# The 64-token tail of the gate's v: high and low part as one stationary factor, 8 matmuls for 12

## Chip, cores and metric

The kernel runs on one core of one Trainium2 chip. The metric is the device time of one execution in microseconds. Three runs of the kernel before gave 655.53, 655.45 and 653.43 us; their median is 655.45.

## What is computed

Three layers follow each other, for a batch of 4, 576 tokens and 512 channels, all in float32:

- attention with 8 heads of 64, each query seeing itself and the 63 keys before it;
- a gated layer: `h = relu(x @ w_in)` with `w_in` of 512 x 1024, split by columns in `u` and `v` of 512 each; `v` normalised per token, mixed over tokens by `w_spatial` (576 x 576), plus a bias, times `u`, then `@ w_out`;
- a mixer: `h = relu(xt @ w_tok1) @ w_tok2` over the tokens, added to x, then `u + relu(u @ w_ch1) @ w_ch2` over the channels, with `w_ch1` of 512 x 1536.

What matters here is the second layer's v:

```python
h = np.maximum(x @ w_in, 0.0)
u, v = (h[..., :d_ff // 2], h[..., d_ff // 2:])
mu = np.mean(v, axis=-1, keepdims=True)
var = np.mean((v - mu) ** 2, axis=-1, keepdims=True)
v_n = (v - mu) / np.sqrt(var + 1e-06)
```

## The kernel before, in words

**Products in three parts.** TensorE multiplies fp32r data, a float32 rounded to fewer bits. To keep the precision every factor is held twice: a high part (the rounded value, written by ScalarE, GpSimd or VectorE into an fp32r tile) and a low part (the value minus its high part). `product` (L1289) then issues three matmuls into one accumulation: high x high, high x low, low x high. The first factor of `pe.matmul` is the stationary one, the second the moving one. `xhl[:, s, k, token]` holds x, transposed, high (s=0) and low (s=1) for the four groups k of 128 channels; `w_in_s[:, s, k, :]` holds w_in.

**Tiles of tokens.** 576 tokens are four tiles of 128 (t = 0 to 3) and a tail of 64 (t = 4). In `gate_values` (L1396) the tokens' x is the stationary factor, 128 columns wide for a tile and 64 for the tail, and 512 columns of w_in move: 4 groups x 3 products = 12 matmuls for each tile, and 12 for the tail as well. `gate_inputs` (u) and `mix_tokens` (g) move 288 columns, half of the tokens, and have eight units each per batch.

**From a finished v.** `relu_v` (L816) on ScalarE takes the ReLU from PSUM into `vr`, which has two halves used in turn, so that tile t shares its half with tile t - 2 and waits for the low part of that tile. `stats` (L1062), `spread` on GpSimd (L693) and `norm` (L1073) normalise it there, `vn_high` (L823) and `normalised_lo` (L1084) write high and low part for the mixing. Of the tail, the low part lies in partitions 64 to 127 of the high part's place, so that the mixing over 64 tokens takes two matmuls instead of three; place 4 of the low half of `vn` is free.

**Banks.** Units v, u, g, y, t, a, b and w take four PSUM banks in turn, the one used longest ago first (L158 to L178). `take_acc` (L1365) waits until the last user's result has been read (`unit_free`, L435): for v, u and y that is a ScalarE operation, for the others one of VectorE.

**Orders.** Every engine and SyncE's queue of transfers works through a list written out by hand, and each is in order. A list has a prologue (attention of batch 0), a first, two equal loops (attention of batches 1 to 3, with the second and third layer of the batch before) and an epilogue. In the list of TensorE Q, K, Z are transposes of q, k and the tail of both, S scores, T transposes of the probabilities, V attention's product with v, w transposes of w_spatial, v, u, g, y the gated layer, t, a, b the token mixer, P the first products of the last layer; "+" is the second half of the unit opened last. ScalarE's `vr`, `vh` are ReLU and high part of v, `uu` the ReLU of u, `e` the exponentials, `o` attention's output; VectorE's `vs`, `vn`, `vl` are statistics, norm and low part; GpSimd's `n` normalises probabilities, `xh`, `xl` split x, `xo`, `ao`, `wo` form low parts for the last layer. SyncE's `lq`, `lk`, `lv`, `lz` load q, k, v and the tail of q and k, `lw` the weights (0: w_in for v, 1: w_in for u, 2: w_spatial, 3: w_out, 4: w_tok1, 5: w_tok2, 6: bias). Loads of q and k go round three slots, so the seventh waits until the fourth slot's transposes are done; v has three places in batch 0, and lv03 waits until V1 is done.

## Time and profile before

| | us |
|---|---|
| median of three runs (lowest, highest) | 655.45 (653.43, 655.53) |
| the profiled execution | 653.59 |
| its span, first to last instruction | 651.0 |
| busy: TensorE / VectorE / ScalarE / GpSimd | 638.4 / 433.1 / 297.8 / 138.4 |
| mean clock granted to TensorE, of full speed | 1.000 |

The page counts an engine as busy while an instruction of its datapath runs. Matmuls overlap: one lasts longer than the distance at which the next one starts, so their price is read from starts, not from durations. In the rows below PE is TensorE, DVE VectorE, ACT ScalarE, POOL GpSimd and SPq the transfers that SyncE issues. "128\*64 128x512" is a matmul with 128 rows and 64 columns of stationary factor and 512 moving columns. In brackets stands the idle time before a group and what ended it; a timeline merges neighbours of one line, and names the shape of the first.

### The profile page before, as it was taken

What the parts mean: (1) busy time and instruction counts of PE and PEld (TensorE: products, weight loads), DVE (VectorE), ACT (ScalarE), POOL (GpSimd) and SP (SyncE); (2) the same over time, 40 slices, a digit from 0 to 9 for tenths busy, and PEclk for the clock granted to TensorE, in tenths of its full rate; (3) what the DMA queues carried; (4) which work ended last, traced back from release to release, by engine and by line L of the source; (5) the groups of instructions that cost most, each with busy time, mean ns of one, the idle gap of its engine ahead of it and who ended that gap; (6) DMA issues with size and microseconds to landing.
All of it is one profiled execution on the core that took longest, in us unless ns stands there. A gap on an engine that the chain in (4) does not pass through costs nothing.

```text
span 651.0 us, 11538 instructions
## 1 busy us (share of the span) xinstructions
PE 638.4 (98%) x3917; PEld 589.1 (90%) x3917; DVE 433.1 (67%) x1073; ACT 297.8 (46%) x733; POOL 138.4 (21%) x232
## 2 busy tenths in 40 slices
PE   5899999999999999999999999999999999999997
PEld 5798999989998899988999989988898889889886
DVE  4988887666865778766473666776756775755534
ACT  4865447334464344652347334453334454243331
POOL 3561426531234304252107700000000000000000
PEclk9999999999999999999999999999999999999999
DMA  9858135586444883344730174252632332422412
GB/s 209 212 92 197 35 86 158 129 169 107 128 117 116 178 139 87 107 121 113 165 128 2 61 177 134 73 173 83 213 108 65 121 107 64 163 64 66 162 33 97
DMA packets 190872, 77.48 MB, mean 119 GB/s; under 512 B 127328, under 2 KB 177056, under 8 KB 190816
## 3 DMA queue, kind: packets, MB, share of 16 engines
q1 hardware_dynamic: 190816, 76.76, 45.2%
q8 instruction: 32, 0.52, 0.3%
q14 instruction: 24, 0.20, 0.1%
HBM read 55.49 MB, written 21.23 MB: 118 GB/s over the span
## 4 chain that ended last, share of the span: by engine, by line
PE 95%; DMA 2%; DVE 1%; POOL 1%; SPq 0%; issue 0%; ACT 0%; POOLq 0%; DVEq 0%
PE ps L1291 71%; PE ps L1392 13%; PE ps L1361 4%; PE ps L1331 4%; DMA early<-in_moe_w_spatial_dram 2%; PE ps L1455 1%; PE ps L1310 0%; PE ps L1380 0%; DMA out_dram<-front 0%; DVE front L1195 0%; PE ps L1341 0%; DVE att L995 0%; ACT att L763 0%; POOL att L675 0%; SPq L544 0%
## 5 line engine op out<-in xcount | busy, mean ns | idle before, releaser
L1291 PE MATMUL ps<-arena 128*128 128x288 f32 (+3 forms) x2100 | 396.3, 342 | 0.0
L1291 PEld LDWEIGHTS ps<-arena 128*128 128x128 f32 (+1 forms) x2100 | 335.2, 186 | 33.7
L1291 PE MATMUL ps<-att_r,arena 128*128 128x384 f32 x504 | 101.5, 336 | 0.0
L1291 PEld LDWEIGHTS ps<-att_r,arena 128*128 128x128 f32 x504 | 90.0, 188 | 7.1
L1392 PE MATMUL ps<-arena 128*128 128x288 f32 (+1 forms) x560 | 89.6, 316 | 0.0
L1392 PEld LDWEIGHTS ps<-arena 128*128 128x128 f32 x560 | 80.5, 188 | 4.1
L690 POOL TENSOR_SCALAR att<-att,rinv 128x128 f32<-128x128 f32 x144 | 53.8, 393 | 98.1 <-DVE rinv L1006 97.9
L783 ACT ACTIVATE att<-att,nmax 128x128 f32<-128x128 f32 x144 | 56.0, 392 | 25.8 <-DVE nmax L995 25.3
L881 ACT ACTIVATE xT<-ps 128x384 f32<-128x384 f32 x54 | 26.5, 491 | 52.1 <-PE ps L1291 52.1
L1171 DVE TENSOR_TENSOR arena<-front,arena 128x1792 fp32r<-128x1792 f32 x16 | 32.4, 2025 | 16.1 <-ACT arena L873 16.0
L1181 DVE TENSOR_TENSOR vr<-ps,xT 128x384 f32<-128x384 f32 x36 | 20.0, 556 | 31.7 <-PE ps L1291 25.0
L995 DVE CUSTOM_DVE_ANT_0 att<-ps,mask 128x128 f32<-128x128 f32 x144 | 33.1, 285 | 11.5 <-PE ps L1331 11.0
L893 ACT ACTIVATE arena<-vr 128x384 fp32r<-128x384 f32 x36 | 18.7, 520 | 43.8 <-PE ps L1291 35.7
L1331 PE MATMUL ps<-att 128*128 128x128 f32 x288 | 37.4, 280 | 0.9 <-DVE att L969 0.9
L1361 PE MATMUL ps<-att 128*128 128x128 f32 x288 | 37.1, 276 | 0.7 <-DVE att L969 0.4
L873 ACT ACTIVATE arena<-front 128x1792 fp32r<-128x1792 f32 x18 | 30.7, 1704 | 13.4 <-DVE front L1161 13.4
L1186 DVE SCALAR_TENSOR_TENSOR arena<-vr,arena 128x384 fp32r<-128x384 f32 x36 | 21.2, 589 | 23.3 <-ACT arena L893 23.3
L1331 PEld LDWEIGHTS ps<-att 128*128 128x128 f32 x288 | 35.4, 196 | 1.3 <-DVE att L969 1.2
L1361 PEld LDWEIGHTS ps<-att 128*128 128x128 f32 x288 | 34.7, 192 | 1.7 <-DVE att L969 0.6
L793 ACT ACTIVATE xT<-ps 64x256 f32<-64x256 f32 x72 | 27.1, 377 | 14.6 <-PE ps L1361 13.6
L893 ACT ACTIVATE arena<-xT 128x384 fp32r<-128x384 f32 x18 | 9.5, 525 | 48.4 <-PE ps L1291 32.7
L1129 DVE TENSOR_TENSOR uy<-ps,uy 128x288 f32<-128x288 f32 x32 | 14.2, 454 | 20.4 <-PE ps L1291 20.3
(101 smaller groups left out, 651.8 us busy)
## 6 DMA issues: line engine op xcount, KB each, us to landing
front<-in_moe_w_ch_dram SPq DMA_DIRECT2D x18, 512.0 KB, 4.7
prob_blocks<-att SPq DMA_DIRECT2D x27, 256.0 KB, 2.5
att<-prob_blocks SPq DMA_DIRECT2D x108, 64.0 KB, 2.0
u_scratch<-uy SPq DMA_DIRECT2D x16, 288.0 KB, 2.9
front<-in_moe_w_ch_dram SPq DMA_DIRECT2D x18, 256.0 KB, 2.9
front<-in_moe_w_ch_dram SPq DMA_DIRECT2D x36, 128.0 KB, 3.5
early<-u_rows SPq DMA_DIRECT2D x18, 256.0 KB, 5.6
att<-in_v_dram SPq DMA_DIRECT2D x16, 256.0 KB, 3.8
```

The costliest lines, as they stand in the source:

```text
L690: ins = pool.tensor_scalar(x, x, rinv[:, g % 3, p:p + 1], 1.0, ALU.mult, ALU.mult)
L783: ins = act.activation(x, x, ACT.Exp, bias=nmax[:, g % 3, p:p + 1], scale=-1.0, accum_out=psums[:, g % 3, p:p + 1])
L793: ins = act.activation(xT3[c, :, blk * WINDOW:(blk + 1) * WINDOW], tp[c, bank, :].rearrange("p (w h n) -> p w h n", w=PAIRS, h=2)[:, :, h, ...
L873: act.activation(a_hi_at[n % 2], a_raw[n % 2], ACT.Copy).then_inc(a_hi, 1)
L881: act.activation(part[x], ps[:, 6, 0:CK], ACT.Copy).then_inc(part_copied, 1)
L893: act.activation(h_at[:, j, 0], total[i], ACT.Relu).then_inc(h_hi, 1)
L995: ins = dve.tensor_tensor_reduce(out=prob[:, g % 3, P * p:P * (p + 1)], in0=ps[:, 4 + g % 2, P * p:P * (p + 1)], in1=mask[:, 0:P] if blk e ...
L1171: dve.tensor_tensor(a_lo_at[n % 2], a_raw[n % 2], a_hi_at[n % 2].bitcast(F32), ALU.subtract).then_inc(a_low, 1)
L1291: ins = pe.matmul(dst, w[a], x[c], start=first and n == 0, stop=last and n == 2, skip_group_check=True)
L1331: ins = pe.matmul(ps[:, 4 + g % 2, P * p:P * (p + 1)], qd[:, g // 2 % 2, g % 2, p].rearrange("p h n -> p (h n)"), kT[:, p, at:at + P], sta ...
L1361: ins = pe.matmul(tp[:, bank, P * p:P * (p + 1)], window[:, P * p:P * (p + 1)], keys[:, p], start=True, stop=True)
L1392: ins = pe.matmul(dst, d, w, start=t == 0 and n == 0, stop=t == NT - 1 and n == len(pairs) - 1, skip_group_check=True)
```

## The change

For the tail, high and low part of x are written beside each other a second time, into `xtail` (128 columns: 64 high, 64 low, at the free place 4 of `vn`). One matmul with these 128 columns against the high part of w_in gives high x high in PSUM rows 0 to 63 and low x high in rows 64 to 127; a second one with the 64 high columns adds high x low to rows 0 to 63. That is 8 matmuls for 12. ScalarE copies rows 64 to 127 to `vtail` in SBUF (`tail_low`, "vt4", on the bytes of `xtail`, which has been read by then), VectorE adds them to rows 0 to 63 and writes `vr` (`tail_sum`, "va4"), ScalarE takes the ReLU in place. The bank is free after `tail_sum`. The engines that split x write `xtail` as well: ScalarE and VectorE in batch 0, GpSimd in the others. All lists of orders are replaced; those that matter below are shown, the list of SyncE with its first lines.

```diff
 ...
     PROLOGUE_PE = (
-        "Q0 K0 Q1 S0 S1 K1 K2 S2 Q2 T0 S3 V0 T1 S4 S5 T2 V1 K3 Q3 V2 T3 S6 S7 V3 T4 w0 w1 v0 Z4 w2 V4 S8 T5 + V5 "
-        "T6 v1 + w3 T7 V6 v2 + u00 V7 T8 + u10 + u20 V8 + u30 + v3 + w4 v4 + u01 w5 + u11 + u21 + u31 +").split()
+        "Q0 K0 Q1 S0 S1 K1 K2 S2 Q2 T0 S3 T1 V0 S4 S5 T2 V1 K3 Q3 T3 V2 S6 S7 V3 T4 w0 v0 w1 Z4 V4 w2 S8 T5 + V5 "
+        "T6 w3 v1 + V6 T7 v2 + u00 V7 T8 + u10 + u20 + V8 u30 + v3 w4 + v4 + u01 + u11 w5 + u21 + u31 +").split()
 ...
     LOOP_PE = (
-        "g00 S0 S1 + g10 S2 S3 + g20 + g30 + g01 + g11 + g21 + g31 S4 S5 V0 V1 + y00 + y10 + y20 + y30 + y01 S6 "
-        "V2 t0 + y11 + y21 + y31 + t1 S7 V3 t2 S8 V4 t3 t4 a0 a1 a2 a3 v0 a4 V5 V6 + v1 + b00 b10 b20 b30 b01 b11 "
-        "V7 V8 b21 v2 + b31 v3 + v4 + u00 + u10 + u20 + u30 + u01 + u11 + u21 + u31 +").split()
+        "g00 S0 S1 + g10 + S2 S3 g20 + g30 + g01 + g11 + g21 + g31 + y00 S4 V0 V1 + y10 + y20 + y30 + y01 S5 V2 "
+        "t0 S6 + y11 + y21 + y31 + S7 t1 V3 t2 t3 t4 S8 V4 a0 a1 a2 v0 a3 a4 V5 V6 + v1 + b00 b10 b20 b30 b01 V7 "
+        "V8 b11 b21 b31 v2 + v3 + v4 + u00 + u10 + u20 + u30 + u01 + u11 + u21 + u31 +").split()
 ...
     EPILOGUE_PE = (
-        "g00 + g10 + g20 + g30 + g01 + g11 + g21 + g31 + y00 + y10 + y20 + y30 + y01 + t0 t1 y11 + y21 + y31 + a0 "
-        "t2 t3 a1 t4 a2 a3 a4 P0 P1 b00 P2 b10 P3 b20 P4 b30 b01 P5 b11 P6 b21 b31").split()
+        "g00 + g10 + g20 + g30 + g01 + g11 + g21 + g31 + y00 + y10 + y20 + y30 + y01 t0 t1 + y11 + y21 + y31 + a0 "
+        "t2 t3 P0 P1 a1 t4 a2 a3 a4 P2 P3 P4 b00 b10 b20 b30 P5 b01 b11 b21 P6 b31").split()
 ...
     LOOP_ACT = (
-        "e0 e1 e2 gh00 gh10 gh20 e3 gh30 gh01 e4 gh11 yy00 o0 o1 yy10 yy20 gh21 gh31 yy30 o2 yy01 th0 e5 yy11 e6 "
-        "yy21 yy31 th1 th2 o3 th3 e7 o4 e8 th4 ah0 o5 ah1 vr0 o6 vr1 vh0 o7 o8 vr2 vh1 vr3 vh2 uu00 vr4 vh3 uu10 "
-        "uu20 uu30 uu01 uu11 vh4 uu21 uu31").split()
+        "e0 e1 gh00 gh10 e2 gh20 gh30 gh01 gh11 e3 e4 yy00 yy10 yy20 gh21 gh31 o0 yy30 e5 yy01 o1 yy11 th0 yy21 "
+        "e6 yy31 th1 o2 th2 th3 e7 th4 o3 e8 o4 ah0 o5 o6 ah1 vr0 vr1 o7 vh0 o8 vr2 vh1 vt4 vh2 vr3 uu00 vr4 uu10 "
+        "vh3 uu20 uu30 vh4 uu01 uu11 uu21 uu31").split()
 ...
     EPILOGUE_DVE = (
-        "sa00 sm00 gl00 sa10 sm10 gl10 sa20 sm20 sa30 gl20 as0 sm30 xs0 gl30 sa01 sa11 sm01 gl01 sm11 sa21 gl11 "
-        "sa31 xs1 sm21 sm31 xs2 gl21 gl31 as1 xs3 tl0 tl1 tl2 tl3 tl4 al0 al1 te00 cs0 te10 dh0 te20 te30 te01 "
-        "cs1 te11 dh1 dh2 cs2 te21 te31 dh3 ut0 ut1 ut2 ut3").split()
+        "xs0 sa00 sa10 sm00 sm10 gl00 sa20 gl10 sm20 as0 sa30 xs1 gl20 sa01 sm30 sm01 gl30 sa11 sm11 gl01 sa21 "
+        "xs2 sm21 gl11 sa31 sm31 gl21 gl31 xs3 tl0 tl1 as1 tl2 tl3 tl4 cs0 al0 al1 dh0 cs1 te00 te10 dh1 te20 "
+        "te30 te01 dh2 te11 te21 cs2 te31 dh3 ut0 ut1 ut2 ut3").split()
 ...
     EPILOGUE_POOL = (
-        "xo0 xo1 ao0 xo2 xo3 ao1 xo4 xo5 xo6 wo0").split()
+        "xo0 ao0 xo1 xo2 xo3 xo4 wo0 xo5 ao1 xo6").split()
 ...
     LOOP_DVE = (
-        "qt0 qt1 qt2 m0 qt3 m1 qt4 m2 r0 qt5 r1 sa00 pt0 sa10 sm00 sm10 pt1 gl00 gl10 sa20 r2 sm20 sa30 m3 gl20 "
-        "sa01 sm30 sm01 m4 gl30 r3 sa11 pt2 sm11 gl01 sa21 gl11 sa31 sm21 sm31 pt3 qt6 vo1 gl21 r4 gl31 m5 pt4 m6 "
-        "tl0 qt7 r5 vo2 qt8 tl1 r6 pt5 tl2 m7 pt6 m8 r7 tl3 tl4 vo3 r8 pt7 al0 pt8 al1 vs0 te00 te10 te20 vo4 "
-        "te30 te01 vn0 vs1 te11 vl0 te21 te31 vn1 ut0 vs2 ut1 vl1 vn2 vs3 vl2 vn3 ut2 ut3 vs4 kt0 vl3 vn4 kt1 vl4").split()
+        "qt0 qt1 qt2 m0 qt3 m1 qt4 r0 m2 r1 pt0 sa00 sm00 sa10 qt5 gl00 sm10 pt1 sa20 gl10 sa30 sm20 sm30 gl20 "
+        "sa01 gl30 r2 sm01 sa11 m3 sm11 gl01 pt2 sa21 gl11 m4 sa31 r3 sm21 qt6 sm31 vo1 r4 pt3 gl21 gl31 m5 qt7 "
+        "pt4 vo2 r5 m6 tl0 qt8 m7 pt5 tl1 r6 tl2 pt6 tl3 m8 vo3 tl4 r7 r8 pt7 pt8 al0 al1 vs0 vn0 te00 te10 te20 "
+        "vo4 te30 vs1 te01 te11 te21 vl0 te31 ut0 ut1 vs2 vn1 vn2 ut2 vl1 kt0 vl2 va4 vs3 kt1 vn3 vs4 ut3 vn4 vl3 "
+        "vl4").split()
 ...
     ALL_SP = (
-        "lq00 lk00 lq01 lv00 lv01 lk01 lq02 lk02 lw01 lq03 lk03 lv02 lw00 lw02 lz04 lv03 lk10 lv04 lq10 lw06 lv10 "
-        "lw03 lv11 lw04 pw10 pr10 pw11 pr11 pw12 pr12 lw05 lv12 pw13 pw14 pr13 pr14 lv13 pw15 pw16 pr15 pr16 lv14 "
 ...
+        "lq00 lk00 lq01 lv00 lk01 lv01 lk02 lq02 lw01 lq03 lv02 lk03 lw00 lw02 lv03 lz04 lw04 lv04 lk10 lw06 lw03 "
+        "lq10 lv10 pw10 pr10 lv11 pw11 pr11 pw12 lw05 pr12 lv12 pw13 pw14 pr13 pr14 pw15 lv13 pw16 pr15 pr16 pw17 "
 ...
@@ -257,6 +258,12 @@
         vn = region("vn").rearrange("p (s t n) -> p s t n", s=2, t=NT)
 
 
+        VT = START["vn"] - START["w_out"] + (2 * NT - 1) * G
+        vtail = early[0:TAIL, VT:VT + G]
+
+        xtail = vn[:, 1, NT - 1, :].rearrange("p (k s n) -> p k s n", k=KD, s=2)
+
+
         def raw(name, n, k):
             at = START[name] - START["w_out"]
             return early[:, at:at + n].rearrange("p (k n) -> p k n", k=k)
@@ -349,6 +356,7 @@
         w2_hi = sem("w2_hi")
         w2_lo = sem("w2_lo")
         a_low = sem("a_low")
+        tail_copied = sem("tail_copied")
         w2_low = sem("w2_low")
         xc_low = sem("xc_low")
         xc_in = [sem(f"xc_in{i}") for i in range(2)]
@@ -414,7 +422,7 @@
 
 
         ACC_ACT = counts(ACT_ORDER, ("vr", "uu", "yy"))
-        ACC_DVE = counts(DVE_ORDER, ("sa", "tl", "al", "te", "wl"))
+        ACC_DVE = counts(DVE_ORDER, ("sa", "tl", "al", "te", "wl", "va"))
         TP_ACT = counts(ACT_ORDER, ("qe", "ze", "o"))
         TP_DVE = counts(DVE_ORDER, ("ke", "c"))
         K_TURNED = counts(DVE_ORDER, ("kt",))
@@ -434,6 +442,8 @@
 
         def unit_free(u):
             kind, b, x = u
+            if (kind, x) == ("v", NT - 1):
+                return acc_dve, ACC_DVE["va", b, x]
             if kind in ("v", "u", "y"):
                 return acc_act, ACC_ACT[{"v": "vr", "u": "uu", "y": "yy"}[kind], b, x]
             return acc_dve, ACC_DVE[{"g": "sa", "t": "tl", "acc_a": "al", "b": "te", "w": "wl"}[kind], b, x]
@@ -701,10 +711,16 @@
                 apart(pool)
                 pool.wait_ge(*unit_full(("y", b - 1, 31)))
                 apart(pool)
+                if t == NT - 1:
+                    apart(pool)
+                    pool.wait_ge(*unit_free(("v", b - 1, t)))
+                    pool.tensor_scalar(xtail[:, :, 0, :], xT3[:, :, toks(t)], 1.0, 1.0, ALU.mult, ALU.mult)
                 pool.tensor_scalar(xhl[:, 0, :, toks(t)], xT3[:, :, toks(t)], 1.0, 1.0, ALU.mult, ALU.mult).then_inc(x_hi_pool, 1)
 
             def x_low(b, t):
                 pool.wait_ge(x_hi_pool, NT * (b - 1) + t + 1)
+                if t == NT - 1:
+                    pool.tensor_tensor(xtail[:, :, 1, :], xT3[:, :, toks(t)], xhl[:, 0, :, toks(t)].bitcast(F32), ALU.subtract)
                 pool.tensor_tensor(xhl[:, 1, :, toks(t)], xT3[:, :, toks(t)], xhl[:, 0, :, toks(t)].bitcast(F32), ALU.subtract) \
                     .then_inc(x_lo_pool, 1)
 
@@ -796,6 +812,8 @@
 
             def x_high(t):
                 act.wait_ge(*use_free("V", 0, last_blk(t)))
+                if t == NT - 1:
+                    act.activation(xtail[:, :, 0, :], xT3[:, :, toks(t)], ACT.Copy)
                 act.activation(xhl[:, 0, :, toks(t)], xT3[:, :, toks(t)], ACT.Copy).then_inc(x_hi, 1)
 
             def spatial_hi(t):
@@ -813,8 +831,19 @@
                                          ACT.Copy)
                 ins.then_inc(sp_hi, 1)
 
+            def tail_low(b):
+
+                if b > 0:
+                    act.wait_ge(*unit_free(("v", b - 1, NT - 1)))
+                act.wait_ge(*unit_full(("v", b, NT - 1)))
+                act.activation(vtail, ps[TAIL:P, BANK_OF["v", b, NT - 1], :], ACT.Copy).then_inc(tail_copied, 1)
+
             def relu_v(b, t):
                 n, r = NT * b + t, rows(t)
+                if t == NT - 1:
+                    act.wait_ge(*unit_free(("v", b, t)))
+                    act.activation(vr[0:r, n % 2, :], vr[0:r, n % 2, :], ACT.Relu).then_inc(acc_act, 1)
+                    return
                 if n >= 2:
                     act.wait_ge(vn_lo, n - 1)
                 act.wait_ge(*unit_full(("v", b, t)))
@@ -905,6 +934,8 @@
                     x_high(x)
                 elif kind == "wh":
                     spatial_hi(x)
+                elif kind == "vt":
+                    tail_low(b)
                 elif kind == "vr":
                     relu_v(b, x)
                 elif kind == "vh":
@@ -1026,6 +1057,8 @@
 
             def x_low(t):
                 dve.wait_ge(x_hi, t + 1)
+                if t == NT - 1:
+                    dve.tensor_tensor(xtail[:, :, 1, :], xT3[:, :, toks(t)], xhl[:, 0, :, toks(t)].bitcast(F32), ALU.subtract)
                 dve.tensor_tensor(xhl[:, 1, :, toks(t)], xT3[:, :, toks(t)], xhl[:, 0, :, toks(t)].bitcast(F32), ALU.subtract) \
                     .then_inc(x_lo, 1)
 
@@ -1059,10 +1092,17 @@
                                             w_sp_s[:, 0, 0:NT - 1, toks(t)].bitcast(F32), ALU.subtract)
                 ins.then_inc(acc_dve, 1)
 
+            def tail_sum(b):
+                n, bank = NT * b + NT - 1, BANK_OF["v", b, NT - 1]
+                dve.wait_ge(vn_lo, n - 1)
+                apart(dve)
+                dve.wait_ge(tail_copied, b + 1)
+                dve.tensor_tensor(vr[0:TAIL, n % 2, :], ps[0:TAIL, bank, :], vtail, ALU.add).then_inc(acc_dve, 1)
+
             def stats(b, t):
                 n, r = NT * b + t, rows(t)
                 i = n % 2
-                dve.wait_ge(*unit_free(("v", b, t)))
+                dve.wait_ge(acc_act, ACC_ACT["vr", b, t])
                 dve.bn_stats(vst[0:r, i, :], vr[0:r, i, :]).then_inc(stats_done, 1)
                 dve.wait_ge(stats_done, n + 1)
                 apart(dve)
@@ -1215,6 +1255,8 @@
                     x_low(x)
                 elif kind == "wl":
                     spatial_lo(x)
+                elif kind == "va":
+                    tail_sum(b)
                 elif kind == "vs":
                     stats(b, x)
                 elif kind == "vn":
@@ -1401,6 +1443,12 @@
                     if b == 0 and t == 0:
                         apart(pe)
                         pe.wait_ge(*piece_lo("v", i))
+                    if t == NT - 1:
+
+                        pe.matmul(acc, xtail[:, i].rearrange("p s n -> p (s n)"), w_in_s[:, 0, i, G:FF], start=i == 0, stop=False, skip_group_check=True)
+                        ins = pe.matmul(acc[0:TAIL, :], xhl[:, 0, i, toks(t)], w_in_s[:, 1, i, G:FF], start=False, stop=i == KD - 1,
+                                        skip_group_check=True)
+                        continue
                     ins = product(acc[0:rows(t), :], [xhl[:, s, i, toks(t)] for s in range(2)],
                                   [w_in_s[:, s, i, G:FF] for s in range(2)], i == 0, i == KD - 1)
                 if part == 1:
```

## Rows read from the trace of the kernel before

**Rows 1.** The page: busy time of the engines, and the granted clock in 40 slices
```profile
PE 638.4 (98%) x3917; PEld 589.1 (90%) x3917; DVE 433.1 (67%) x1073; ACT 297.8 (46%) x733; POOL 138.4 (21%) x232
...
PEclk9999999999999999999999999999999999999999
```

**Rows 2.** Windows of the start and of the last layer: busy us (instructions), clock, DMA share, GB/s
```profile
10.00:30.00 20.00, 16.29 (x129) 14.39 (x128) 17.63 (x83) 16.20 (x65) 9.77 (x22) 1.00 1.01 253
360.00:644.00 284.00, 284.00 (x1431) 256.02 (x1430) 177.41 (x270) 114.54 (x173) 9.82 (x5) 1.00 0.34 107
```

**Rows 3.** The chain that ended last: start us, us, engine and line, count
```profile
38.60 2.78 PE ps L1291 x12
```

**Rows 4.** Groups by line and shape, TensorE: count, busy us, mean ns
```profile
L1291 PE MATMUL ps<-arena 128*64 128x512 f32 x48 | 11.7, 393 | 0.0
```

**Rows 5.** Timeline of TensorE, three short looks at batch 3: start us, us, count
```profile
306.61 0.61 PE L1291 MATMUL ps<-arena 128*128 128x512 f32 x2
...
307.07 0.40 PE L1291 MATMUL ps<-arena 128*64 128x512 f32 x1
...
309.83 0.42 PE L1291 MATMUL ps<-arena 128*128 128x288 f32 x2
```

**Rows 6.** Groups by line and shape, ScalarE and VectorE, 64 partitions by 512
```profile
L821 ACT ACTIVATE vr<-ps 64x512 f32<-64x512 f32 x4 | 2.3, 587 | 3.5 <-PE ps L1291 1.8 <-DVE arena L1087 1.7
...
L1118 DVE TENSOR_TENSOR arena<-ps,arena 64x512 fp32r<-64x512 f32 x4 | 2.7, 684 | 5.5 <-ACT arena L849 5.5
```

**Rows 7.** Timeline of TensorE in batch 3, from b21 to the mixing
```profile
299.88 22.83 PE L1291 MATMUL ps<-arena 128*128 128x288 f32 x144
322.54 1.74 PE L1392 MATMUL ps<-arena 128*128 128x288 f32 x12
```

**Rows 8.** Timelines in batch 3: ScalarE after u31, VectorE's low part of tile 2
```profile
322.82 0.41 ACT L834 ACTIVATE uy<-ps 128x288 f32<-128x288 f32 x1 [1.19 <-PE ps L1291]
...
310.48 0.68 DVE L1087 TENSOR_TENSOR arena<-vr,arena 128x512 fp32r<-128x512 f32 x1
```

**Rows 9.** Timeline of GpSimd in batch 3: high and low part of the tail
```profile
302.54 0.41 POOL L704 TENSOR_SCALAR arena<-xT 128x256 fp32r<-128x256 f32 x1
303.03 0.73 POOL L708 TENSOR_TENSOR arena<-xT,arena 128x256 fp32r<-128x256 f32 x1
```

**Rows 10.** Timeline of TensorE at the start: T4, w0 with w1, Z4
```profile
29.07 0.66 PE L1341 MATMUL ps<-ident,att 128*128 128x128 f32 x4
30.05 1.09 PE L1380 MATMUL ps<-ident,early 128*128 128x128 f32 x8 [0.33 <-DMA early<-in_moe_w_spatial_dram]
...
32.37 0.60 PE L1310 MATMUL ps<-ident,att 128*128 128x128 f32 x4
```

**Rows 11.** Timeline of SyncE's queue at the start: issue us, us
```profile
15.66 0.37 SPq L530 DMA_DIRECT2D att<-in_k_dram  x1
16.07 0.58 SPq L539 DMA_DIRECT2D att<-in_v_dram  x1
...
19.54 1.41 SPq L527 DMA_DIRECT2D att<-in_k_dram  x1
22.71 2.04 SPq L539 DMA_DIRECT2D att<-in_v_dram  x1
```

**Rows 12.** DMA issues at 18.2 and 19.5 us: KB, us to landing
```profile
early<-in_moe_w_spatial_dram SPq DMA_DIRECT2D x1, 144.0 KB, 11.8
...
att<-in_k_dram SPq DMA_DIRECT2D x1, 128.0 KB, 11.4
```

**Rows 13.** Timelines at the last layer's start: GpSimd's low parts, then TensorE
```profile
346.44 3.64 POOL L721 TENSOR_TENSOR att_r<-att,att_r 128x768 fp32r<-128x768 f32 x2 [30.87 <-DVE att L1151]
350.02 4.08 POOL L728 TENSOR_TENSOR arena<-front,arena 128x1792 fp32r<-128x1792 f32 x1
...
353.15 1.64 PE L1392 MATMUL ps<-arena 128*128 128x512 f32 x6
...
358.73 2.27 PE L1291 MATMUL ps<-att_r,arena 128*128 128x384 f32 x12
```

More of the change, by code:

```diff
@@ L62, in bass_attention_gmlp_mixer_kernel @@
-        "y11 + S6 V2 t0 y21 + t1 S7 y31 + a0 t2 t3 V3 S8 t4 V4 v0 a1 a2 a3 a4 + V5 V6 b00 b10 b20 b30 v1 + b01 "
-        "b11 b21 V7 V8 v2 + b31 v3 + v4 + u00 + u10 + u20 + u30 + u01 + u11 + u21 + u31 +").split()
+        "g00 + g10 S0 + g20 + S1 S2 g30 + g01 S3 + g11 + g21 + g31 + y00 V0 S4 S5 + y10 + y20 + y30 + y01 V1 S6 "
+        "t0 t1 + y11 V2 + y21 + y31 + a0 t2 t3 V3 S7 t4 V4 S8 a1 a2 a3 v0 a4 + V5 V6 b00 b10 b20 v1 + b30 b01 b11 "
+        "V7 v2 V8 + b21 b31 v3 + v4 + u00 + u10 + u20 + u30 + u01 + u11 + u21 + u31 +").split()
@@ L76, in bass_attention_gmlp_mixer_kernel @@
-        "yy21 th1 yy31 o2 th2 th3 o3 th4 o4 e7 e8 ah0 ah1 vr0 vh0 o5 vr1 o6 o7 o8 vr2 vh1 vr3 vh2 vr4 uu00 uu10 "
-        "vh3 vh4 uu20 uu30 uu01 uu11 uu21 uu31").split()
+        "gh00 e0 gh10 e1 e2 gh20 gh30 e3 gh01 gh11 yy00 yy10 yy20 o0 gh21 gh31 yy30 e4 th0 o1 yy01 th1 e5 yy11 "
+        "yy21 yy31 e6 th2 o2 o3 th3 o4 e7 th4 e8 ah0 ah1 o5 o6 vr0 vr1 o7 vh0 o8 vr2 vh1 vr3 vt4 vh2 vr4 vh3 uu00 "
+        "uu10 uu20 vh4 uu30 uu01 uu11 uu21 uu31").split()
     LOOP_ACT = (
-        "e0 e1 e2 gh00 gh10 gh20 e3 gh30 gh01 e4 gh11 yy00 o0 o1 yy10 yy20 gh21 gh31 yy30 o2 yy01 th0 e5 yy11 e6 "
```

24 lines of the change are left out of this document (11 added, 13 removed), and 16 rows, old and new, of tables (ALL_SP, FIRST_DVE).

## Prediction

> **What bounds the kernel now.** I read the page first: TensorE is busy for 638.4 of 651.0 us, VectorE for 433.1, and the clock granted to TensorE is 9 tenths of full speed or more in all forty slices [rows 1]. A busy share alone does not settle it, since matmul ends are modelled, so I looked for gaps stage by stage: from 360 to 644 us the engine is busy for 284.0 of 284.0 us, from 10 to 30 us for only 16.29 of 20 [rows 2]. TensorE is full from about 34 us until its last products, and the only stretch with air in it is the start. That gives two rules. A matmul removed after 34 us is worth its full spacing. A changed order on another engine is worth nothing there, unless it makes TensorE wait; at the start it can shift the whole kernel either way.
>
> **The price of a matmul.** Twelve 128-wide matmuls over 512 columns advance the chain by 2.78 us, 0.232 each [rows 3]. Do those whose stationary factor has only 64 columns go faster? There are 48, the tail's twelve in each of four batches, 393 ns long on average [rows 4]. In batch 3 two 128-wide ones start at 306.61, the tail's twelve run from 307.07 on, and at 309.83 the 288-column ones begin: 0.46 / 2 = 0.230 before the tail and 2.76 / 12 = 0.230 in it [rows 5]. The spacing follows the moving columns, not the width of the stationary factor. So a factor of 128 columns costs no more than one of 64 did, and 8 matmuls take 1.84 us for 2.76.
>
> **Part 1, the removal.** (12 - 8) x 0.230 = 0.92 us per batch, times 4 batches: **-3.7 us**, all of it on the path. The weight loads that go too count as nothing: they lie beside the matmuls.
>
> **Part 2, ScalarE's copy and VectorE's sum.** ScalarE gets one more operation per batch, a 64x512 copy out of PSUM, 587 ns by the present ReLU of this shape; the ReLU then reads SBUF, which I take at the same. VectorE gets a 64x512 sum out of PSUM, 684 ns by the low part of the same shape [rows 6]. What counts is when the bank of v4 comes free. It took one ScalarE operation, now it takes two on two engines, and the sum also waits for the low part of tile 2, which holds the same half of vr. The bank is next taken by u30. In batch 3 the 96 matmuls of the u units fill 309.83 to 322.54, 1.59 us a unit [rows 5, 7]. With the tail over at 309.83 - 0.92 = 308.9, u30 opens at 308.9 + 3 x 1.59 = 313.7. A ScalarE operation starts 0.28 us after the next unit's start (322.54, 322.82 [rows 7, 8]), so the copy ends at 308.9 + 0.28 + 0.59 = 309.8. The low part of tile 2 ran from 310.48 for 0.68 us [rows 8], to 311.2; the sum then ends at 311.9. Slack: 1.8 us. Queued behind the copy on ScalarE are the high part of tile 2 and the ReLU of tile 3, whose bank u20 wants at 312.1: with 0.6 each they end at 311.0, slack 1.1. Queued behind the sum on VectorE are the statistics of tile 3; the mixing needs what follows from them only in its second part, after 322.54 [rows 7]. Cost: 0, covered by these slacks; without them each microsecond late is one microsecond per batch.
>
> **Part 3, GpSimd's second copy of the tail's high and low part** (batches 1 to 3; in batch 0 ScalarE and VectorE make it). Operations of this shape take 0.41 and 0.73 us, the last one ending at 303.76 [rows 9]; with 1.14 more it is 304.9, where the tail's matmuls start at 307.07 [rows 5]. Slack 2.2 us, cost 0. Parts 2 and 3 together are bounded by 0 and some 1 us per batch, if a slack proves an illusion because engines slow each other; nothing in them can gain. I take 0, as the slacks are the nearest rows.
>
> **Part 4, the new orders at the start.** TensorE has 3.7 us of air between 10 and 30 us [rows 2]: that bounds the gain. The last piece of it is plain: the fifth probability transposes begin at 29.07 and the next matmuls, the transposes of the spatial weights, at 30.05, waiting for their transfer [rows 10]; four transposes more or less are 1.09 - 0.66 = 0.43, so the engine could have begun at 29.5. That transfer is issued behind the third v load. SyncE stood until 15.66 for a free q/k slot, issued k, and v at 16.07 for 0.58 us [rows 11]. The new order puts this v ahead of k, into the idle stretch, so the spatial weights go out 0.6 us sooner with 256 KB less before them. Their 144 KB part took 11.8 us to land [rows 12]; it should now land a microsecond or more before 30.0. Moved the other way: lv01 goes behind lk01 and lq02 behind lk02 on SyncE's queue, both wanted microseconds later, and w_tok1 goes in front of the k load of batch 1, which waits for the scores anyway. The likely gate is then the transposes at 29.5 instead of 30.05: 0.5, a little more if these move up too, a little less if T1 before V0 and T3 before V2 trade one wait for another. I take **-0.6 us**, between -2 (half of the air) and +1.
>
> **Part 5, the new orders at the end of the batches.** The first two products of the last layer move ahead of a1, from 358.73 to where a1 began, 353.15. They need GpSimd's low part of the weights, which ended at 350.02 + 4.08 = 354.1, behind two low parts of data of 1.82 each [rows 13]. The new GpSimd order has it behind one: 352.3, slack 0.9, and more since VectorE now forms the sums of data that GpSimd waits for before those of the weights. Cost 0; bounds 0 and 0.9, what would be missing without either.
>
> **Sum.** -3.7 - 0.6 = -4.3 us. The profiled execution took 653.59 us (span 651.0), which gives 649.3. The median of the three runs is 655.45, the lowest 653.43: the profiled one lies 1.9 under the median. I put the change against the median: 655.45 - 4.3 = **651.2 us**.
>
> **Rivals.**
> (a) *Width changes empty the array.* Today the tail has two changes of stationary width, in and out, and the spacing across both is the ordinary one [rows 5]. The new tail alternates 128 and 64 columns: seven changes inside and one out, 8 for 2, 24 more in all. If each cost what a matmul lasts beyond its spacing, 0.40 - 0.23 = 0.17 us, that is 4.1: 655.45 - 4.3 + 4.1 = **655.3 us**, no change. For it: no row has a change inside one accumulation. Against: rows 5. Chance 0.04. The Trainium skill, TensorEngine Tiling (Array Packing), Key Properties, says that changing the tiling mode drains TensorE; if 64 columns count as another mode, this rival is what the rule gives. The trace disagrees where it has such a boundary.
> (b) *The bank of v3 or v4 comes free late.* If the slacks of 1.1 and 1.8 us are lost in the in-order queues of ScalarE (copy, tile 2, tile 3) or VectorE, by 1 us in three batches, it is 651.2 + 3 = **654.2 us**. Chance 0.06, of it 0.02 for less than that.
> (c) *Slower: the tail of q and k lands late.* Its second load was issued at 19.54 and landed 11.4 us later, at 30.9, for a use at 32.37 [rows 10 to 12]. Both now stand behind lv03, issued at 22.71 for 2.04 us because it waits for V1 [rows 11], so the second goes out at about 25.4. With 11.4 us again it lands at 36.8, and w_tok1, now issued right behind, shares its engines: 576 KB at the 253 GB/s of this stretch [rows 2] are 2.3 us more, 39.1. TensorE, in order, stands 39.1 - 32.4 = 6.7 us at Z4: 655.45 - 3.7 + 6.7 = **658.5 us**. It makes the kernel slower once the landing comes after 36.1. Against: most of the 11.4 us was the queue ahead, which was empty by then; I estimate a landing at 31. Chance 0.10, half for the full price, 0.04 for a part that ends within 0.3%, 0.01 for less.
> (d) *The change isn't what it says*: the products left out can be counted in the diff. Chance nil.
>
> **Chances.** 0.3% of 655.45 is 2.0 us, about what a measurement of this kernel can tell from no change. The forecast has 0.80. Faster: 0.80 + 0.02 + 0.01 = 0.83. Same: 0.04 of (a), 0.04 of (b), 0.04 of (c) = 0.12. Slower: 0.05. The range reaches from a start that gains 2 and a run among the lowest, 655.45 - 3.7 - 2.0 - 1.4 = 648.4, up to 653.9, nearly to (b).
>
> **What the profile after would show.** Right: 16 fewer matmuls; the tail's eight spaced 0.23; no wait of TensorE from 34 us to the last products; the spatial transposes at about 29.5. Wrong: a wider spacing at the alternating matmuls (a); TensorE idle ahead of u20 or u30, released by ScalarE or VectorE (b); idle ahead of Z4, released by the q or k transfer (c); a wait of the last layer's first products for GpSimd (part 5).

## The result, and the profile after

The changed kernel takes **664.56 us** (median of 6 runs, 663.45 to 666.18) where the kernel before takes 653.08 (6 runs, 651.71 to 655.53): ratio 1.0169, 95% interval 1.0143 to 1.0196. It is 11.5 us slower. The forecast was 651.2 us, between 648.4 and 653.9, which is 4.3 less than the 655.45 that three runs of the kernel before had given; six runs put that kernel at 653.08, so on this base the same change would be 648.8. Every run of a kernel is told with the kernel before on the same chip, whose medians lie between 653.08 and 653.29.

The page after: busy time, and TensorE with its granted clock in 40 slices of 16.6 us.

```profile
span 662.5 us, 11528 instructions
PE 636.7 (96%) x3901; PEld 589.0 (89%) x3901; DVE 446.2 (67%) x1078; ACT 300.4 (45%) x738; POOL 141.5 (21%) x238
...
PE   5899999999999999999999929999999999999997
...
PEclk9999999999999999999999969999999999999999
```

3901 matmuls for 3917 [rows 1], busy 1.7 us less, and still a span 11.5 us longer. One slice of forty, from 380.9 to 397.5 us, has TensorE at 2 tenths and its clock at 6. The waits of TensorE name the place:

```profile
PE ps L1333 <- ACT xT L910: 12.4, 3, 11.6
```

The chain through it (start us, us, what), from the stores to TensorE:

```profile
383.95 0.52 SPq L593
...
384.56 0.48 SPq L605
...
385.66 3.11 DMA front<-in_moe_w_ch_dram
388.79 0.42 DVE front L1196
...
389.92 0.43 DVE front L1201
390.40 1.57 issue
391.98 0.48 ACT xT L910
...
392.60 2.69 PE ps L1333 x7
```

L593 are the sixteen stores of the last batch's transposed rows ("sr30" to "sr33"), L605 to L607 the load of the third piece of the last layer's weights ("ca42"). SyncE, an in-order queue, reaches it only when the last store has gone. VectorE forms the sums of the weights (L1196 to L1201), ScalarE their high part (L902, 1.6 us, in the "issue" of 390.40) and, behind that in its own queue, the copy L910 that frees TensorE's bank. Before, the load stood ahead of the stores. SyncE in the last layer's first stage, before and then after (start us, us):

```profile
373.64 0.41 SPq L595 DMA_DIRECT2D front<-in_moe_w_ch_dram  x1
...
375.22 7.29 SPq L583 DMA_DIRECT2D u_rows<-early  x12
382.56 2.21 SPq L583 DMA_DIRECT2D u_rows<-gate  x4
...
388.40 0.47 SPq L595 DMA_DIRECT2D front<-in_moe_w_ch_dram  x1
```

```profile
371.16 2.33 SPq L593 DMA_DIRECT2D u_rows<-early  x4
...
375.12 7.09 SPq L593 DMA_DIRECT2D u_rows<-early  x8
382.26 2.20 SPq L593 DMA_DIRECT2D u_rows<-gate  x4
384.56 0.48 SPq L605 DMA_DIRECT2D front<-in_moe_w_ch_dram  x1
```

Third weights at 373.64 before, at 384.56 after. TensorE runs dry at 381 and begins again at 392.60, at the lower of its clock's levels. Windows of it (busy us and count of PE, PEld, DVE, ACT, POOL; clock, DMA share, GB/s):

```profile
388.00:392.00 4.00, 0.00 (x0) 0.00 (x0) 1.52 (x4) 1.62 (x2) 0.00 (x0) 0.50 0.96 302
...
395.00:396.00 1.00, 1.00 (x4) 0.73 (x3) 0.81 (x2) 0.53 (x2) 0.00 (x0) 0.55 0.00 0
396.00:397.00 1.00, 1.00 (x7) 0.87 (x6) 1.00 (x2) 0.00 (x0) 0.00 (x0) 1.00 0.00 0
```

The ledger, read at the same 384-column matmul of both traces:

| at (before, us) | after minus before | what lies between |
|---|---|---|
| 372.50 | -3.18 | start and four batches |
| 384.01 | +8.59 | the stand of 11.62 |
| 386.44 | +10.18 | clock at 0.50 until nearly 396 |
| 478.15 | +10.58 | 0.4 at a wait (idle for 0.22 of it) |
| 638.35 | +11.41 | 0.75 at a wait (idle for 0.53 of it), and rest |

So the gain was there until 372 us, and one transfer took back more than four times as much.

Each lead has about 1 us of scatter in it, since the kernel before stands in it as one execution. That one begins batch 3's gates (g00) at 322.54; the executions of Experiments 2 and 7 below, whose programs are the same up to there, begin them at 321.53 and 322.16.

### The profile page after: what moved, and what is told of

The parts are those of the page before. It is cut to its first block, busy times and chain, and to the rows that moved or that the text cites. A ratio compares the mean times of both kernels' runs of the same rounds, so it can differ in the third digit from the quotient of the medians.

```text
span 662.5 us, 11528 instructions
## 1 busy us (share of the span) xinstructions
PE 636.7 (96%) x3901; PEld 589.0 (89%) x3901; DVE 446.2 (67%) x1078; ACT 300.4 (45%) x738; POOL 141.5 (21%) x238
## 4 chain that ended last, share of the span: by engine, by line
PE 86%; DMA 4%; SPq 3%; DVE 3%; ACT 2%; issue 1%; POOL 1%; DVEq 0%; POOLq 0%; ACTq 0%
PE ps L1333 61%; PE ps L1434 13%; PE ps L1403 4%; PE ps L1373 4%; DMA front<-in_moe_w_ch_dram 2%; SPq L593 2%; PE ps L1503 1%; DMA early<-in_moe_w_in_dram 1%; DVE front L1235 1%; DMA prob_blocks<-att 1%; PE ps L1449 1%; PE ps L1448 1%; PE ps L1352 0%; ACT att L799 0%; DVE arena L1215 0%
## 5 line engine op out<-in xcount | busy, mean ns | idle before, releaser
L1333 PE MATMUL ps<-arena 128*128 128x512 f32 (+2 forms) x2052 | 386.6, 341 | 0.2 <-ACT xT L910 0.2
L1333 PEld LDWEIGHTS ps<-arena 128*128 128x128 f32 x2052 | 329.0, 188 | 30.1 <-issue 0.6
L1434 PEld LDWEIGHTS ps<-arena 128*128 128x128 f32 x560 | 80.5, 188 | 4.0
L910 ACT ACTIVATE xT<-ps 128x384 f32<-128x384 f32 x54 | 26.4, 489 | 50.1 <-PE ps L1333 50.1
L902 ACT ACTIVATE arena<-front 128x1792 fp32r<-128x1792 f32 x18 | 30.7, 1705 | 28.0 <-DVE front L1201 28.0
L1026 DVE CUSTOM_DVE_ANT_0 att<-ps,mask 128x128 f32<-128x128 f32 x144 | 33.1, 286 | 12.2 <-PE ps L1373 11.5
L1055 DVE STREAM_TRANSPOSE att<-att 128x512 f32<-128x512 f32 x27 | 19.2, 711 | 18.6 <-PE ps L1403 16.2
```

Of the source, the lines that this page charges most:

```text
L902: act.activation(a_hi_at[n % 2], a_raw[n % 2], ACT.Copy).then_inc(a_hi, 1)
L910: act.activation(part[x], ps[:, 6, 0:CK], ACT.Copy).then_inc(part_copied, 1)
L1026: ins = dve.tensor_tensor_reduce(out=prob[:, g % 3, P * p:P * (p + 1)], in0=ps[:, 4 + g % 2, P * p:P * (p + 1)], in1=mask[:, 0:P] if blk e ...
L1333: ins = pe.matmul(dst, w[a], x[c], start=first and n == 0, stop=last and n == 2, skip_group_check=True)
L1434: ins = pe.matmul(dst, d, w, start=t == 0 and n == 0, stop=t == NT - 1 and n == len(pairs) - 1, skip_group_check=True)
```

## The experiments

**Theories.** A: the third weights behind the sixteen stores are the loss. B: the new tail, or the new orders of the computing engines, delay the last layer. C, formed for what A would leave: the start of the last layer is a second bound, through SyncE's queue (last b results, transposes, sixteen stores, their landing, data, fourth weights), so that what TensorE gains ahead of it is given back there. D: the fourth weights' transfer is slow whatever stands ahead of it.

An experiment's interval reaches 1.0 to 1.3 us to either side (2.1 in Experiment 2), so a difference of about 1 us between two experiments counts here only where their traces show where it comes from.

**Experiment 1, the third weights early, in the changed kernel** (e1_ca42_early)

```diff
-        "ca41 st30 st31 sr30 st32 cw41 st33 sr31 sr32 sr33 ca42").split()
+        "ca41 st30 st31 ca42 sr30 st32 cw41 st33 sr31 sr32 sr33").split()
```

> The changed kernel with one entry of SyncE's list moved: ca42 (the third weights of the last layer) ahead of sr30 instead of behind sr33. Theory A (the transfer behind four stores that wait for VectorE's last transposes, TensorE stalled 11.6 us through ScalarE's in-order queue): TensorE's long wait near 380 us is gone, no slow clock behind it, and the time is the 3.7 us of the removed matmuls less 0.25 at the start and less 0.4 to 1.5 in small waits: 2 to 3.5 us under the kernel before. Theory B (the new tail, or the new lists of the compute engines, make the last layer late): a wait of 8 us or more stays, and the kernel is 6 to 11 us over the kernel before.

654.51 us (12 runs), ratio 1.0015 (0.9997 to 1.0033). One token takes back 10 of the 11.5 us. But the 3.2 us of gain stay away: the 2 to 3.5 us under the kernel before that theory A expected were missed. A wait of 3.8 us is left, one piece of weights later:

```profile
387.14 2.11 SPq L600 DMA_DIRECT2D early<-u_scratch  x3
...
389.80 0.47 SPq L605 DMA_DIRECT2D front<-in_moe_w_ch_dram  x1
...
400.40 2.26 PE L1333 MATMUL ps<-att_r,arena 128*128 128x384 f32 x6 [3.81 <-ACT xT L910]
...
396.58 0.43 DVE L1196 TENSOR_TENSOR front<-front 128x256 f32<-128x256 f32 x1 [6.07 <-DMA front<-in_moe_w_ch_dram]
```

That execution was the slowest of its twelve (657.36), so 3.8 is a bad case of this wait, not its mean.

**Experiment 2, the third weights late, in the kernel before** (e2_before_ca42_late)

```diff
-        "cw40 cw41 st30 st31 st32 st33 ca42 sr30 sr31 sr32 sr33").split()
+        "cw40 cw41 st30 st31 st32 st33 sr30 sr31 sr32 sr33 ca42").split()
```

> The kernel before with the one entry ca42 moved behind sr33, nothing else. Theory A: the load goes out at about 384.8 us instead of 373.6, TensorE stands 8 to 11 us for it and another 1.5 us go to the lower clock after the stand: 9 to 13 us slower than the kernel before. Theory B: no more than 1 us slower.

664.46 us (4 runs), ratio 1.0152 (1.0119 to 1.0184), as theory A expected, with the stand at the same place. TensorE comes there 4.0 us later than in the changed kernel (385.00 for 380.97), so the stand is 3.7 us shorter:

```profile
392.95 2.26 PE L1291 MATMUL ps<-att_r,arena 128*128 128x384 f32 x6 [7.94 <-ACT xT L881]
```

A is shown both ways: the token alone makes the loss, and taking it away removes most of it.

**Experiment 3, the new tail in the lists of before** (e3_old_orders_new_tail): the tail's code as in the changed kernel, and of the lists nothing but "vt4" and "va4" put in. ScalarE's loop list, for one:

```diff
-        "yy21 yy31 th1 th2 o3 th3 e7 o4 e8 th4 ah0 o5 ah1 vr0 o6 vr1 vh0 o7 o8 vr2 vh1 vr3 vh2 uu00 vr4 vh3 uu10 "
+        "yy21 yy31 th1 th2 o3 th3 e7 o4 e8 th4 ah0 o5 ah1 vr0 o6 vr1 vh0 o7 o8 vr2 vh1 vr3 vh2 uu00 vt4 vr4 vh3 uu10 "
```

> The eight-matmul tail with its copy and sum, in the lists of the kernel before (vt4 put ahead of vr4, va4 on VectorE behind vl2, nothing else moved). Theory A: 16 matmuls of 0.23 us go and nothing else happens, 3 to 4 us faster than the kernel before, no TensorE wait after 34 us. Theory B in the form that the new tail makes engines late: no gain, or slower.

651.66 us (12 runs), ratio 0.9967 (0.995 to 0.9983): faster than before, by 1.6 us, half of the 3 to 4 expected. The tail is no cost, so B falls for the tail. In its trace it leads by 3.9 us when the last layer begins and by 1.7 at the end; between lie VectorE's wait for the fourth weights and TensorE's for a bank:

```profile
393.71 0.43 DVE L1195 TENSOR_TENSOR front<-front 128x256 f32<-128x256 f32 x1 [3.86 <-DMA front<-in_moe_w_ch_dram]
...
397.53 1.28 PE L1332 MATMUL ps<-att_r,arena 128*128 128x384 f32 x6 [1.60 <-ACT xT L909]
```

In the kernel before, VectorE had this wait too, and TensorE none:

```profile
395.64 0.42 DVE L1156 TENSOR_TENSOR front<-front 128x256 f32<-128x256 f32 x1 [1.86 <-DMA front<-in_moe_w_ch_dram]
```

**Experiment 4, the new orders with the old tail** (e4_new_orders_old_tail): Experiment 1 without the tail's edit.

```diff
-        "vl2 va4 vn3 vs4 kt0 vn4 vl3 ut3 kt1 vl4").split()
+        "vl2 vn3 vs4 kt0 vn4 vl3 ut3 kt1 vl4").split()
...
-                if t == NT - 1:
-                    pe.matmul(acc, xtail[:, i].rearrange("p s n -> p (s n)"), w_in_s[:, 0, i, G:FF], start=i == 0, stop=False, skip_group_check=True)
```

> The twelve-matmul tail of the kernel before in the new lists, with ca42 ahead of sr30. It leaves out the copy and the sum. Theory A: the other new orders are worth between a gain of 0.3 and a loss of 1.5 us (0.25 at the start and up to 1.2 of small waits in the changed kernel's trace). Theory B in the form that the new lists of the compute engines are at fault: 6 us or more slower.

657.58 us (10 runs), ratio 1.0053 (1.0033 to 1.0072), with a TensorE wait of 3.0 us for L882, the same copy. The tail is worth 657.58 - 654.51 = 3.1 us under these orders. The orders themselves, third weights early, cost 4.3 us against before. That misses both expectations, A's (at most 1.5) and B's (6 or more). The trace puts all of it behind batch 3's gates: they begin at 321.51, 1.0 us ahead of the kernel before, and the last 384-column matmul is 3.5 us behind (641.84 for 638.35). Between lie that wait and, at the lower clock after it, 1.4 us on eighteen matmuls (401.78 to 406.68, 4.9 us for 3.5). So B holds for the orders at the end of the lists.

**Experiment 5, the landing of the stores not waited for** (e5_e3_stores_unwaited). In Experiment 3 SyncE waits, ahead of the data that it loads after the last store, for the landing of all stores of batch 3, which only later data read. The wait is moved to those.

```diff
-                sp.wait_ge(u2_stored[m], 16 * B)
-                sp.wait_ge(rows_stored[m], 64 * B)
+                sp.wait_ge(u2_stored[m], 16 * (B - 1))
...
+                if n == 4:
+                    for m in range(KD):
+                        sp.wait_ge(u2_stored[m], 16 * B)
+                        sp.wait_ge(rows_stored[m], 64 * B)
```

> The new tail in the old lists, and SyncE no longer waits for the landing of batch 3's stores ahead of the next data and the fourth weights of the last layer (it waits for batches 1 and 2 there, and for all ahead of the first load that reads what they stored). Theory C (the last layer's start is bounded by SyncE's queue as well: load, sixteen stores, their landing, data, fourth weights; the kernel before just met it, and each microsecond that TensorE arrives sooner is given back): the wait of 1.6 us near 397 us goes, and the time is 3 to 4 us under the kernel before instead of 2.2. Theory D (the transfer itself is slow there whatever is ahead of it, 5.7 to 7.2 us from issue to landing): no change against the run without this edit, 1.5 to 2.5 us under the kernel before.

650.33 us (12 runs), ratio 0.9952 (0.9937 to 0.9968): 3.0 us, C's side of the expectation. The long waits of VectorE and TensorE are gone, and the lead stays nearly whole: -3.25 us at the start of the last layer, -2.84 at its end. SyncE, in Experiment 3 and here:

```profile
378.38 2.21 SPq L592 DMA_DIRECT2D u_rows<-gate  x4
383.44 1.40 SPq L599 DMA_DIRECT2D early<-u_scratch  x3
```

```profile
379.08 2.22 SPq L592 DMA_DIRECT2D u_rows<-gate  x4
381.52 1.65 SPq L599 DMA_DIRECT2D early<-u_scratch  x3
```

Between last store and data lie 2.8 us in the first and 0.2 in the second.

**Experiment 6, the same edit on Experiment 1** (e6_e1_stores_unwaited)

> The changed kernel with ca42 ahead of sr30 and SyncE's wait for the stores' landing moved back. Theory C: most of the 3.8 us wait and of the 2 us lost behind it to the lower clock go, 2 to 4 us faster than the kernel before. Theory D: as without this edit, 0.5 to 1.5 us slower than the kernel before.

652.13 us (12 runs), ratio 0.9988 (0.997 to 1.0005), 2.4 us less than Experiment 1, but 1.2 under the kernel before where C wanted 2 to 4. TensorE still waits 1.9 us in three pieces for L913: with the new end of the lists the last store is over at 383.7, against 381.3 in Experiment 5.

**Experiment 7, the same edit on the kernel before** (e7_before_stores_unwaited)

> The kernel before with SyncE's wait for the stores' landing moved back and nothing else. Theory C: TensorE did not wait there, so 0 (within 1 us), with VectorE's wait of 1.9 us for the fourth weights shorter or gone. Theory D: 0 too, but VectorE's wait stays.

653.19 us (10 runs), ratio 0.9991 (0.9975 to 1.0008): nothing, though VectorE's wait of 1.86 us is gone (the sums begin at 393.31, right behind the operation before). This is the control that C needs. The earlier landing is worth nothing in the old kernel. With the new tail it is worth 1.3 us in the medians (Experiment 5 against 3), which is near their noise, and in the traces it takes away TensorE's wait of 1.60. It became a bound only when TensorE arrived sooner. Against this control the new tail is worth 653.19 - 650.33 = 2.9 us.

**Experiment 8, the fourth weights ahead of the data** (e8_e3_weights_ahead_of_data), on Experiment 5:

```diff
-                if n == 1:
+                if n == 2:
...
-                if n in (1, NI):
+                if n in (2, NI):
```

> As the new tail in the old lists with the landing not waited for, and the four loads of data for the next third also behind the fourth and fifth weights instead of ahead. Theory C: the fourth weights go out as soon as their buffer is free, 3.5 to 4 us faster than the kernel before, unless the data then come late for VectorE's sums (then 1 to 3 us are lost 8 to 10 us later). Theory D: no better than 2.2 us.

651.63 us (12 runs), ratio 0.9981 (0.9962 to 0.9999): no better, 1.3 us worse. From issue to landing the 256 KB piece of the fourth weights takes 6.0 us in Experiment 3 and 2.9 here:

```profile
front<-in_moe_w_ch_dram SPq DMA_DIRECT2D x1, 256.0 KB, 6.0
```

```profile
front<-in_moe_w_ch_dram SPq DMA_DIRECT2D x1, 256.0 KB, 2.9
```

But now the data come late, and TensorE waits 1.4 us for VectorE behind them:

```profile
395.80 0.96 DVE L1185 TENSOR_TENSOR early<-xT,early 128x768 f32<-128x768 f32 x1 [4.04 <-DMA xT<-u_scratch]
```

D falls with Experiment 5's time and with these two rows (the time alone, 1.7 us under the kernel before, would have suited D too): what counts is a transfer's place in the queue, and whichever of the two is second is late.

**Experiment 9, the changed kernel with the old end of all lists** (e9_old_end_of_lists): its start and loops kept, every list from the last batch's b results on as before. SyncE's, for one:

```diff
-        "pr35 pr36 pw37 pw38 lv34 pr37 pr38 cx40 cx41 st20 st21 cx42 st22 sr20 sr21 sr22 st23 sr23 cx43 ca40 cw40 "
-        "ca41 st30 st31 sr30 st32 cw41 st33 sr31 sr32 sr33 ca42").split()
+        "pr35 pr36 pw37 pw38 lv34 pr37 pr38 st20 cx40 st21 sr20 st22 cx41 sr21 st23 sr22 sr23 cx42 ca40 ca41 cx43 "
+        "cw40 cw41 st30 st31 st32 st33 ca42 sr30 sr31 sr32 sr33").split()
```

> The changed kernel, start and loops of batches kept, but with the end of every engine's list (from the last batch's b results on) in the order of the kernel before, the third weights early among them. Theory C (the start of the last layer is a second bound that SyncE's queue sets, through the last b results, the sixteen stores and their landing; the new order of the end feeds it later): like the kernel with the old orders and the new tail, 1 to 3 us faster than before, a wait of TensorE of 1 to 2.5 us between 395 and 400 us, SyncE's last store ending near 381 us. Rival (the new start and the new loops are what cost the rest): 0 or slower than before, with the lead over the kernel before already smaller than 3 us at 350 us.

652.86 us (12 runs), ratio 0.999 (0.9973 to 1.0007). A miss for C, which wanted 1 to 3 us and a wait of 1 to 2.5: it is 1.65 us less than Experiment 1, but 1.2 more than Experiment 3, and TensorE's longest wait there is 0.6 us. The trace leads by only 1.74 us when the last layer begins, on the rival's side, but that lead has the 1 us of scatter in it.

**Experiment 10, Experiment 9 with the landing not waited for** (e12_old_end_unwaited; the edit of Experiment 5)

> As the previous one, and SyncE does not wait for the landing of the last batch's stores until the data that read them are due. Theory C: 2.5 to 4 us faster than before, no wait of TensorE over 0.5 us between 380 and 405 us. Rival (new start and loops cost): over 1 us slower than the kernel with the old orders, the new tail and the same unwaited stores (0.9952 of before).

651.77 us (11 runs), ratio 0.9965 (0.9948 to 0.9983), 1.4 us more than Experiment 5. By its time that is the rival's side again. The traces do not show it. Batch 3's gates begin at (us, one execution each):

| start and loops | old tail | new tail |
|---|---|---|
| as before | 321.53, 322.16, 322.54 (Experiments 2 and 7, before) | 318.61, 319.05, 319.29, 319.41 (Experiments 3, 8, 5, 12) |
| new | 321.51 (Experiment 4) | 319.32, 319.36, 319.43, 320.36, 320.81 (Experiments 6 and 1, after, Experiments 10 and 9) |

With the new tail the new lists are 0.8 us later in the mean, with the old tail they are no later, and within one field, where the programs are the same up to there but for a few entries of SyncE's list, the executions lie up to 1.5 us apart. So a cost of the new start and loops is not shown. Part of Experiment 10's own time is a wait of TensorE of 1.6 us at 369.45 for VectorE, which Experiment 5 does not have; the last section shows it.

**Experiment 11, my part 4 by itself** (e10_v2_ahead_of_k3), on Experiment 5:

```diff
-        "lq00 lk00 lq01 lv00 lv01 lk01 lq02 lk02 lw01 lq03 lk03 lv02 lw00 lw02 lz04 lv03 lk10 lv04 lq10 lw06 lv10 "
+        "lq00 lk00 lq01 lv00 lv01 lk01 lq02 lk02 lw01 lq03 lv02 lk03 lw00 lw02 lz04 lv03 lk10 lv04 lq10 lw06 lv10 "
```

> The kernel with the old orders, the new tail and the unwaited stores (0.9952 of before), and one more edit: the third v quarter of the input weights is loaded ahead of the fourth k quarter. If part 4 of the prediction holds by itself, v0 starts 0.3 to 0.6 us earlier and the time is 0.3 to 0.6 us less, 0.9943 to 0.9948 of before. Rival (the landing of z, or the engines between, end the wait there): v0 within 0.1 us, ratio within 0.1 per cent of 0.9952.

649.73 us (9 runs), ratio 0.9946 (0.9928 to 0.9964). The interval holds both answers. In the trace the second part of the spatial weights goes out at 17.58 instead of 18.27, and their transposes start at 29.28 without a wait, where Experiment 5 has 29.85 after 0.34 of waiting:

```profile
29.28 1.04 PE L1424 MATMUL ps<-ident,early 128*128 128x128 f32 x8
```

That looks like the 0.5 us of part 4, and is not evidence for it. Of the seven executions with TensorE's old start and without this move (Experiment 12 has two other loads moved), four have the wait (before 0.33, Experiment 7 0.43, Experiment 5 0.34, Experiment 12 0.70) and three have none: Experiments 2, 3 and 8 start at 29.22, 29.26 and 29.14. A gain from this move alone is not shown.

**Experiment 12, the other two moves of the start** (e11_v1_q2_later), on Experiment 5:

```diff
-        "lq00 lk00 lq01 lv00 lv01 lk01 lq02 lk02 lw01 lq03 lk03 lv02 lw00 lw02 lz04 lv03 lk10 lv04 lq10 lw06 lv10 "
+        "lq00 lk00 lq01 lv00 lk01 lv01 lk02 lq02 lw01 lq03 lk03 lv02 lw00 lw02 lz04 lv03 lk10 lv04 lq10 lw06 lv10 "
```

> The same kernel (0.9952 of before) with the second v quarter moved behind the second k quarter and the third q quarter behind the third k quarter, the other two moves of the change's start. If the late landing of the u quarter is what took back the gain of the start, the u quarter lands over 1 us later and the first TensorE step after it waits 0.2 to 1 us; time 0.2 to 1 us more. Rival (they cost nothing): ratio within 0.1 per cent of 0.9952.

650.32 us (5 runs), ratio 0.9949 (0.9929 to 0.9969): no cost. The u quarter's first cast waits for it until 17.25 instead of starting at 16.83, not a microsecond later. So these two moves do not explain why the new start shows no gain. With all three moves together SyncE is held for 1.77 to 2.41 us by the k load ahead of this quarter (Experiment 5: 0.37), and the cast starts at 17.68 to 18.14 (after, Experiments 1, 6, 9 and 10); with the old tail (Experiment 4) it is 1.17 and 16.50. Whether that costs anything stays open.

## Why the prediction was wrong, point by point

**The step that failed is part 5, "the new orders at the end of the batches", cost 0, bounds 0 and 0.9.** I followed P0 and P1 on TensorE and the low parts on GpSimd, and both did as said: P0 starts at 350.05 without a wait. I did not follow SyncE's queue through the end of its list, though the text of the change had it; I showed only its first lines. Its last line moves one load from ahead of sixteen stores of some 0.6 us each to behind them: 10.9 us later (373.64, 384.56). The view that would have told it is the timeline of SyncE between 368 and 390 us of the kernel before: the load, then 9.5 us of stores. The last of the transposes that they store is over at 376.28 there, and the stores run until 384.77: what they cost is that each holds the queue for 0.5 us or more. How little air this stage had can be read in the same trace: ScalarE's copy, behind the fourth weights in its queue, ends at 399.31, and TensorE takes that bank at 399.69; in Experiment 3, where TensorE waits for this copy, 0.15 us lie between the two. That is some 0.2 us of air.

```profile
398.84 0.47 ACT L881 ACTIVATE xT<-ps 128x384 f32<-128x384 f32 x1
```

```profile
399.69 1.21 PE L1291 MATMUL ps<-att_r,arena 128*128 128x384 f32 x6
```

What the moved load cost, by Experiments 1 and 2, is 10.1 and 11.2 us in the medians (the second without the new tail's lead). The rest of the new end of the lists, which I had also put at nothing, cost another 1.7 in the medians (Experiment 1 against 9).

**Part 1** was right in mechanism and nearly in size. The eight matmuls are spaced 0.22 to 0.24:

```profile
304.86 0.39 PE L1448 MATMUL ps<-arena 128*128 128x512 f32 x1
305.08 0.40 PE L1449 MATMUL ps<-arena 128*64 128x512 f32 x1
...
306.71 2.01 PE L1333 MATMUL ps<-arena 128*128 128x288 f32 x14
```

(306.71 - 304.86) / 8 = 0.231. From gates to gates a batch takes 85.04 to 85.06 us before and 84.14 to 84.17 in Experiments 3 and 5 (one batch of Experiment 3 took 84.52): some 0.9 of the 0.92. What the first batch gave can't be read, as its scatter is as large. In the medians the tail is worth 2.9 to 3.1 us, not 3.7 (Experiments 5 against 7, 1 against 4). With the old orders and the old waits only 1.6 arrive (Experiment 3). "A matmul removed after 34 us is worth its full spacing" holds until the next stage that another queue feeds just in time. How much is given back there I can't tell exactly: C alone would have Experiment 1 gain less over Experiment 4 than the 3.1 it does. My first rule read a busy TensorE as proof that nothing else was near.

**Part 2** was right. ScalarE's copy, VectorE's sum and ScalarE's ReLU in batch 3:

```profile
306.97 0.59 ACT L839 ACTIVATE early<-ps 64x512 f32<-64x512 f32 x1 [1.61 <-PE ps L1449]
...
309.67 0.63 ACT L845 ACTIVATE vr<-vr 64x512 f32<-64x512 f32 x1 [0.66 <-DVE vr L1100]
...
308.95 0.68 DVE L1100 TENSOR_TENSOR vr<-ps,early 64x512 f32<-64x512 f32 x1
```

The copy ends 0.85 us after the tail (foretold 0.87), the sum 2.9 (3.0), each with the durations taken, 0.59 and 0.68. No wait of TensorE there, so rival (b) did not come.

**Part 3** was right: GpSimd's last low part ends at 302.10, the tail starts at 304.86.

```profile
301.36 0.74 POOL L724 TENSOR_TENSOR arena<-xT,arena 128x256 fp32r<-128x256 f32 x1
```

**Part 4** was wrong. The spatial weights do not go out 0.6 us sooner but 0.8 later (the second part at 18.98 instead of 18.21): the k load ahead of them holds SyncE for 1.79 us (15.65 to 17.44), where it took 0.37 before. They still land in time, and the engine comes to them no earlier, at 30.33 for 30.05 [rows 10], having waited elsewhere:

```profile
21.37 0.66 PE L1383 MATMUL ps<-ident,att 128*128 128x128 f32 x4 [0.99 <-POOL att L700]
...
26.25 1.13 PE L1403 MATMUL ps<-att 128*128 128x128 f32 x8 [0.94 <-ACT att L779]
...
30.33 0.60 PE L1422 MATMUL ps<-ident,early 128*128 128x128 f32 x4
```

Nor was the wait that I meant to take away a fixed one: it is in four of seven executions with the old start (Experiment 11). I had read its 0.33 us off a single trace.

**The rivals.** (a) fell by the spacing: by its price the eight would have been 0.17 apart more. The Trainium skill, TensorEngine Tiling (Array Packing), Key Properties, says that a changed tiling mode drains TensorE. The spacing of 0.22 to 0.24 shows no drain at the boundaries of 128 and 64 columns, so by that rule they are no change of mode; no other mode was tried. (c) did not come in the changed kernel, by luck: Z4 began at 32.65 without a wait, but the second of its loads landed at 32.58, where I had estimated 31, so 0.07 us were to spare. In Experiment 9, with the same start, it landed at 33.46 and Z4 waited 0.23. None of my rivals was the one that came, and the slower side had 5 in 100. The rival that should have stood there: a load moved behind stores, with the stores' 9.5 us as its price.
